# SyncE's loads of the prologue and of block 0, each queued behind the landing of an earlier load

## What is computed

```python
# q, k, v: (4, 8, 576, 64); pooled by 4 along the sequence, and a band of +-3
q_d = q.reshape(B, H, Sd, factor, D).mean(axis=3)          # k_d, v_d likewise
out_up = np.repeat(sm_attn(q_d, k_d, v_d), factor, axis=2)
mask = np.abs(pos[:, None] - pos[None, :]) < factor
out_local = softmax(where(mask, scale * q @ k.T, -1e9)) @ v
x = (out_up + out_local)     # as 2304 tokens x 512
h = x @ w_in                 # w_in: 512 x 2048
g = h * np.tanh(log1p(exp(h)))
out = g @ w_out              # w_out: 2048 x 512
```

## Time and profile before

| | us |
|---|---|
| three timed runs | 510.19, 510.17, 505.64 |
| their median | 510.17 |
| the profiled execution | 505.87 |
| its span, first to last instruction | 504.1 |
| busy in it: PE | 487.2 (97%) |
| DVE, ACT, POOL | 219.1, 176.0, 121.2 |
| moved by DMA | 35.01 MB |

### The profile page before, as it was taken

One profiled execution on the slowest core, in us unless ns is written; L12 is line 12 of the kernel. 1 busy time (PEld: TensorE's weight loads), 2 busy tenths in 40 slices (PEclk: granted clock), 3 DMA queues, 4 the chain that ended last, 5 costly groups with the idle time before them and its releaser, 6 DMA issues.

```text
span 504.1 us, 9597 instructions
## 1 busy us (share of the span) xinstructions
PE 487.2 (97%) x4040; PEld 434.7 (86%) x4040; DVE 219.1 (43%) x390; ACT 176.0 (35%) x399; POOL 121.2 (24%) x164
## 2 busy tenths in 40 slices
PE   7789999999999999899999989999999999999997
PEld 7678888988999988788898978989899998999996
DVE  5845875665322234536356363644222222232221
ACT  4664865462211123534353452534121111211111
POOL 3997546524100003134141322412000000000000
PEclk9989999999999999999999999999999999999999
DMA  8995522131200001503213051220010000100001
GB/s 283 334 315 160 203 74 59 48 106 34 89 1 0 1 2 47 169 1 106 59 48 105 3 168 37 70 59 1 1 62 1 0 1 0 44 21 1 0 2 62
DMA packets 15836, 35.01 MB, mean 69 GB/s; under 512 B 1840, under 2 KB 1968, under 8 KB 15792
## 3 DMA queue, kind: packets, MB, share of 16 engines
q1 hardware_dynamic: 15792, 34.38, 21.5%
HBM read 29.66 MB, written 4.72 MB: 68 GB/s over the span
## 4 chain that ended last, share of the span: by engine, by line
PE 86%; issue 3%; DVE 3%; ACT 3%; DMA 2%; POOL 2%; SPq 0%; ACTq 0%; POOLq 0%; DVEq 0%
PE acc L600 38%; PE hidden L583 36%; PE att L478 2%; PE att L491 2%; PE att L537 2%; PE att L507 1%; PE att L544 1%; PE att L519 1%; DMA k_t<-in_k 1%; DMA out<-stage 1%; POOL prob L381 1%; DMA v_win<-in_v_win 1%; POOL prob_pool L389 1%; DVE x_low L802 1%; PE hidden L537 1%
## 5 line engine op out<-in xcount | busy, mean ns | idle before, releaser
L814 DVE CAST g_high<-hidden 128x384 fp32r<-128x384 f32 x96 | 53.4, 557 | 205.3 <-PE acc L600 160.0
L583 PE MATMUL hidden<-x_high,w_in_high 128*128 128x384 f32 x384 | 130.2, 339 | 0.5 <-DVE g_low L816 0.5
L583 PE MATMUL hidden<-x_high,w_in_low 128*128 128x384 f32 x384 | 129.4, 337 | 0.0
L583 PE MATMUL hidden<-x_low,w_in_high 128*128 128x384 f32 x384 | 128.9, 336 | 0.0
L1006 ACT ACTIVATE hidden<-hidden 128x384 f32<-128x384 f32 x96 | 45.7, 476 | 234.2 <-PE hidden L583 233.9
L600 PE MATMUL acc<-w_out_high,g_high 128*128 128x512 f32 x288 | 115.0, 399 | 0.0
L600 PE MATMUL acc<-w_out_high,g_low 128*128 128x512 f32 x288 | 113.4, 394 | 0.0
L600 PE MATMUL acc<-w_out_low,g_high 128*128 128x512 f32 x288 | 113.3, 393 | 0.0
L583 PEld LDWEIGHTS hidden<-x_high,w_in_high 128*128 128x128 f32 x384 | 72.1, 188 | 4.8 <-DVE g_low L816 0.8
L583 PEld LDWEIGHTS hidden<-x_low,w_in_high 128*128 128x128 f32 x384 | 72.1, 188 | 3.1
L583 PEld LDWEIGHTS hidden<-x_high,w_in_low 128*128 128x128 f32 x384 | 72.0, 188 | 0.0
(11 more groups left out here) (93 smaller groups left out, 452.6 us busy)
## 6 DMA issues: line engine op xcount, KB each, us to landing
v_win<-in_v_win SPq DMA_DIRECT2D x16, 384.0 KB, 4.2
v_in<-in_v SPq DMA_DIRECT2D x16, 320.0 KB, 3.6
k_t<-in_k SPq DMA_DIRECT2D x16, 292.0 KB, 3.8
q_t<-in_q SPq DMA_DIRECT2D x16, 288.0 KB, 2.8
out<-stage SPq DMA_DIRECT2D x17, 256.0 KB, 2.1
w_in_raw<-in_w_in SPq DMA_DIRECT2D x16, 256.0 KB, 12.5
w_out_raw<-in_w_out SPq DMA_DIRECT2D x16, 256.0 KB, 5.0
out<-last_stage SPq DMA_DIRECT2D x1, 256.0 KB, 2.1
```

The lines of the kernel that those rows point to most:

```text
L583: last = nc.tensor.matmul(hidden[:, g % HB, 0:TB], w, x[:, k, cols], start=(k == 0 and i == 0), stop=(k == KT - 1 and i == 2))
L814: nc.vector.tensor_copy(g_high[:, g % GB], x).then_inc(g_rounded, 1)
```

## The change

SyncE's list in the prologue and in block 0 keeps its loads and their order. Between them now stand waits for earlier loads: most issues wait until the load three places ahead of it has landed (a load_qk or a load_v counting as one), so that three or four calls are under way at a time. From w_in(7) on it is the load three pieces back. The rest of SyncE's list and all other engines' lists are as they were.

```diff
--- before.py
+++ after.py
@@ -286,25 +286,43 @@
                 sp.dma_start(const[:], const_l).then_inc(const_loaded, 16)
                 load_w_in(0)
                 load_qk(0)
+                sp.wait_ge(const_loaded, 16)
                 load_w_in(1)
+                sp.wait_ge(w_in_loaded[0], 16)
                 load_w_out(0)
+                sp.wait_ge(qk_loaded[0], 32)
                 load_qk(1)
+                sp.wait_ge(w_out_loaded[0], 16)
                 load_qk(2)
+                sp.wait_ge(qk_loaded[1], 32)
                 load_w_in(2)
+                sp.wait_ge(qk_loaded[2], 32)
                 load_v(0)
+                sp.wait_ge(w_in_loaded[2], 16)
                 load_v(1)
+                sp.wait_ge(v_loaded[0], 32)
                 load_qk(3)
+                sp.wait_ge(v_loaded[1], 32)
                 load_w_in(3)
                 load_w_in(4)
+                sp.wait_ge(qk_loaded[3], 32)
                 load_qk(4)
+                sp.wait_ge(w_in_loaded[3], 16)
                 load_w_in(5)
+                sp.wait_ge(w_in_loaded[4], 16)
                 load_w_out(1)
+                sp.wait_ge(qk_loaded[0], 64)
                 load_v(2)
+                sp.wait_ge(w_in_loaded[5], 16)
                 load_w_out(2)
+                sp.wait_ge(v_loaded[2], 32)
                 load_v(3)
+                sp.wait_ge(w_out_loaded[2], 16)
                 load_v(4)
+                sp.wait_ge(v_loaded[3], 32)
                 load_w_in(6)
                 for f in range(7, FT):
+                    sp.wait_ge(w_in_loaded[f - 3], 16)
                     load_w_in(f)
                 sp.wait_ge(out_ready, AHEAD)
                 for f in range(EARLY_OUT, 6):
```

## The result

| | before | after |
|---|---|---|
| timed runs | 9 | 9 |
| median, us | 508.40 | 512.48 |
| lowest and highest, us | 505.64, 510.97 | 511.69, 514.84 |
| profiled execution, us | 505.87 | 512.26 |
| its span | 504.1 | 510.5 |

The ratio of after to before is 1.0086, with a 95% interval of 1.0053 to 1.0119. The change made the kernel slower, by 0.5 to 1.2%. The forecast was 503.3 us and its range ended at 510.3: the sign was wrong and the time lies outside the range.

A forecast was written before the change was run, and what follows sets the result against it. Before 41.15 us the prologue, a chain through all engines, was taken as the bound, then PE itself. Late loads +0.4, stalls -0.7 and -1.6, clock -0.6 gave -2.5 us; added to the profiled 505.87: 503.3 us, range 501.6 to 510.3.

The forecast's parts named there:

- The step that failed: SyncE's list: the waits delay only further loads; w_in(15) goes out at about 41 us, w_out(3) at 41.4.
- (a): Prologue: loads issued later, qk(1), v(0) and qk(3) close to their consumers; POOL passes on +0.4 us (bounds 0 and 1.2).
- (b): Prologue: PE's code refills find a short queue, both "issue" stalls (1.69 and 1.31 us) go: -0.7 and -1.6 us.
- The rule weighed in the prediction: Code refills: DMA engines alternate queues packet by packet, so a shorter backlog gives nothing: 506.3 us.
- The prediction's own rule: Code refills at PE's block ends: the refill lets all queued loads pass, 0.7 MB meaning 2 us of transfer.
- piece of fixed size: Rival 1's reason: the refill stands behind a fixed-size piece of the queue, which four loads may still fill.
- The clock, -0.6 us: Prologue, 35 to 40 us: without PE's stalls the clock does not fall; -0.6 us, 0 if it falls anyway.
- The sum: At outputs(3): +0.4 - 0.7 - 1.6 - 0.6 = -2.5 us, start 37.15 instead of 39.65, kept to the end.
- Rival 3: Prologue, starved queue: qk(1), v(0), qk(3) land late, POOL passes on about 1.5 us, clock falls, 1.0; 508.4 us; chance 0.10.
- Rival 4: Prologue: the clock falls nowhere and the first stall is worth its full 1.69 us: 502.3 us; chance 0.07.
- Rival 1: Prologue: refills wait as long as before, only late loads count: 506.3 us, or 510.6 beside higher runs; chance 0.20.
- Rival 2: Whole kernel: the gain is made, but runs stay at the higher level: 510.2 - 2.5 = 507.7 us; chance 0.23.

The follow-up runs named there:

- e12: Before with only the load of qk(5) moved from behind w_out(5) to behind w_out(15), no wait added: 513.91 us, ratio 1.0129 to before.
- e10: e7 plus two early waits, for qk(0) ahead of w_in(2) and for qk(1) ahead of v(1): 505.67 us, ratio 0.9953 to before.
- e8: Before with its loads in e7's order by need, but without any added wait: 507.95 us, ratio 1.0001 to before.
- e9: After with its 17 single waits, w_in(10) to w_in(15) moved behind w_out(3) and around qk(5): 508.46 us, ratio 1.0022 to before.
- e1: After without the nine waits in the loop over w_in(7) to w_in(15): 509.39 us, ratio 1.0027 to before.
- e5: After with all its waits, only qk(5) moved ahead of w_out(3) to w_out(5): 509.52 us, ratio 1.0044 to before.
- e3: After without its first seven waits, so loads up to v(1) issue freely: 512.67 us, ratio 1.0088 to before.
- e2: Before plus only the nine waits in the loop over w_in(7) to w_in(15): 508.31 us, ratio 1.0000 to before.
- e7: Before with loads reordered by need, free up to v(1), then waits for the load two or three back: 504.65 us, ratio 0.9943 to before.
- e4: Before plus only after's first seven waits, up to v(1): 508.07 us, ratio 1.0002 to before.
- e6: Before with each load waiting for the landing six calls back, where after mostly takes three: 506.72 us, ratio 0.9988 to before.

## Why the prediction was wrong, step by step

**The step that failed.** "Queued behind SyncE's waits are only further loads; w_in(15) now goes out at about 41 us, and w_out(3) right behind it, at 41.4 instead of 41.3". w_in(15) went out at 47.56 and w_out(3) at 47.94. Two things were wrong in it. First the time: each wait was priced at an idle queue's landing (3.1 to 3.8 us) only where a consumer stood close behind it, and the rest of the list was taken to keep up. In the trace the waits stand in series. Predicted and measured landings drift apart: k(1) 10.1 to 10.3 and 10.7; qk(2) 11.6 and 13.3; v(0) 15.9 and 17.9; qk(3) 20.2 and 21.6; qk(4) 23.5 and 27.1; v(2) 27.7 and 32.6; v(3) 32 and 37.3; w_in(6) 35 and 41.5. Second, "only further loads": one of them, qk(5), had a time by which it was wanted. The prediction looked for consumers of late loads up to ACT and w_out(3) and stopped there. A row of before already had POOL idle for 2.75 us in front of this very load, and what stood behind it had hardly any slack: POOL waited another 0.24 us (for DVE) before prob(4), and PE took prob(4) without a gap. The prediction names no row of POOL past 41 us.

**"From there on PE is bound by itself ... so the 2.5 us stay to the end"** was wrong for the same reason. PE was 98% busy after 41.15, but pair 4's and pair 5's chains run under block 0, and they were just in time. e12 shows it without any wait added: 5 us of a load's landing, 7 us of time. Over the kernels of the table b0 stays at 84 us while k(5) is 8.7 or less. Where the block ran at a clock of 1.00, it grows from there by about 1 us for each (e10: 9.6 and 85.56; e8: 9.7 and 84.83; e9: 10.0 and 85.24; e1: 11.2 and 86.92; e5: 12.2 and 87.83), and PE's gap ahead of pair 4's turn grows with it (0.47, 0.56, 0.88, 2.56, 3.22 us). After, e3 and e12 lie above that by the clock's part. e2 and e7 don't belong to the row: no gap, and the clock made both numbers.

**(a) The late loads, +0.4 us** for qk(1), v(0) and qk(3): e4 has the seven waits that make qk(1) and v(0) late, alone, and gives 1.0002; qk(3) landed at 21.6, and POOL took it at 22.26 without waiting. The median shows no such cost, though it can't tell 0.4 us from nothing. POOL's wait for k_t(1) was 1.73 us, as forecast. What was left out is qk(2): pool_q(2) stands ahead of prob(0) in POOL's list, and PE waited 1.40 us for prob(0) instead of 0.66. Beside it v(2), which the prediction gave 1 us of room, landed 4.9 us later than it said; PE lost 1.15 us for it. PE's timeline of after, and POOL's ahead of it:

```profile
34.88 1.23 PE L562 MATMUL hidden<-prob_pool_t,v_pool 72*64 72x144 f32 x8 [1.15 <-POOL v_pool L393]
```
```profile
32.63 0.72 POOL L390 TENSOR_TENSOR v_pool<-v_in 72x256 f32<-72x256 f32 x1 [1.93 <-DMA v_win<-in_v_win]
```

**(b) The stalls, -0.7 and -1.6 us.** Right as far as the stalls go. After has no gap put down to "issue" at the two block ends where before had 1.69 and 1.31 us; only that before outputs(3), 0.59 us, is left, as in before (0.73). e7 against e8 measures the term with all that hangs on it, the clock too: 3.3 us.

**Why the refill is sooner.** At the block end of about 440 (439 instructions had started by 21.16 in after) the refill packet came at about 23.8. Windows of after up to that block end, and the DMA queues of after from 23.7 to 23.9:

```profile
0.00:21.16 21.16, 16.51 (x219) 15.09 (x220) 11.44 (x28) 10.22 (x28) 10.90 (x22) 0.92 0.78 242
```
```profile
q8 instruction: 1, 0.02, 30.5%
```

That is 2.6 us, with three loads of 0.8 MB not yet landed. Counted in the same way before's wait is 4.7 us, with 3.6 MB (the prediction's 4.3 takes the block end 0.4 us too late), and at the later block end with nothing queued 0.6 (the prediction's 0.3). The rule weighed in the prediction ("DMA: Bandwidth & Descriptors" of the Trainium skill, queues, rings and completion order: each engine takes turns between its queues, packet by packet) would have the refill wait for no backlog; the runs speak against it, 0.6 us with nothing queued, 0.9 to 3.6 us with 0.7 to 0.9 MB (after, e7), 3.9 to 6.2 us with 2 MB and more (both profiles of before, e6, e8). The prediction's own rule, that all of the backlog has to pass, is no better at the upper end: 2.0 MB (e6) gave 4.03 us and 3.8 MB (before) 5.51. That is nearer to the rival's "piece of fixed size", except that four loads do not fill it: after's waits are shorter, and its stalls are gone.

**The clock, -0.6 us.** Wrong. From 32 to 41 us the granted clock of after is 0.65, as before's 0.66 from 35 to 40, and it was 0.50 from 18 to 21 us as well (0.88 over the prologue). PE stood still before the first fall for POOL (1.40 us for prob(0), until 17.75) and before the second for POOL's v_pool(2) (1.15 us, until 34.88), rather than for its code. But after's waits don't force this: with the same seventeen waits e9, e5 and e1 ran the prologue at 1.00 and took 40.42 to 41.55 us.

**The sum.** The -2.5 us at outputs(3) didn't come. The forecast put outputs(3) at 37.15, before had it at 39.65, and PE's timeline of after has it here:

```profile
42.26 0.91 PE L555 MATMUL acc<-prob_t,v_win 54*64 54x48 f32 x48 [0.59 <-issue]
```

With the same seventeen waits and the clock at 1.00 it came at 39.71 (e1), 39.02 (e5) and 38.93 (e9), against 39.65 and 41.09 in the two profiles of before. So the stalls' gain was there but smaller than 2.5 us, since PE waited longer for prob(0) and for v(2), and in after's profile the clock took more than all of it. Why after's clock is lower than theirs stays open.

Block 0 adds 3.5 us in the profiles, for the late qk(5): 2.1 of idle time and 1.4 of busy time at the lower clock behind the gap. How much of the 4.1 us between the medians is qk(5) alone is not settled. e1 and e5 keep the gap (2.56 and 3.22 us) and lie only 1.1 and 1.5 us above before. But the clock alone doesn't make the loss either: 66 runs of before, made beside the experiments, had a mean granted clock of 0.987 to 0.993, and the slowest took 510.62 us; the eight runs of after in that range took 511.69 to 514.84.

In the prediction's own figures, the forecast's lower bound of 502.2 doesn't follow from the bounds named beside it (late loads at 0 instead of +0.4 give 503.0), and the sum was added to 505.87, the profile's time, where the median of nine runs is 508.4.

**The rivals.** Rival 3, the starved queue, had the right sign and roughly the right sentence ("each issued only when an earlier one has landed"), but its place was wrong: it looked at qk(1), v(0) and qk(3), none of which cost a time that can be measured, and it would be decided "once qk(1) lands after about 11 us"; qk(1) landed at 10.7. Its fall of the clock behind a wait of PE is in after's profile (0.50 from 18 to 21 us), but not in those of e1, e5 and e9 with the same waits. Rival 4, a clock that falls nowhere, is not what after's runs show: their mean granted clock is 0.983 to 0.993. Rival 1 (the refill waits as before) falls with e7 and e8. Rival 2 was right in one point: the runs of before at 510 exist, and the nine runs' median is 508.4, not the 505.9 of the profile to which the sum was added.

## What to carry to other kernels

A queue's issuing engine is a list like any other: a wait in it delays everything behind it, so follow the last load that the list still has to issue to the time when it is wanted, and look there for an engine that already waits for it (here POOL, idle for 2.75 us in front of k_t(5)). Throttling loads by "wait for the third one back" puts landings in series into that list (after's w_in(6) to w_in(15) took from 37.31 to 47.56 to go out, e1's from 38.44 to 43.54); what paid here was ordering the loads by the time they are wanted together with waits only where the queue would otherwise hold megabytes (e7, ratio 0.9943, where the order alone gave 1.0001 and after's waits alone 1.0086). And a bound engine that is 98% busy is not yet safe from a chain that runs beneath it without slack.

## What the runs showed of the hardware

- The wait of an instruction refill behind the loads under way was 0.6 us with none, 0.9 to 3.6 with 0.7 to 0.9 MB, 4.0 with 2 MB, and 3.9 to 6.2 us with 2.6 to 4 MB, where it no longer grew with the amount. PE went on 1.3 to 1.5 us after the packet's end wherever it was held by it.
- The load of k_t(5), 292 KB, took 3.1 to 3.7 us where one or two other loads had not landed at its issue (both profiles of before, e2, e4, e6, e7), 4.6 to 5.4 with three to five (e5, e8, e9, e10, after) and 5.7 to 6.4 with six to nine (e1, e3, e12). What is issued just ahead of a load that is wanted matters as much as its own issue time.
- The scatter of 2 to 5 us between runs of one kernel goes in part with the granted clock: e5's five runs with a mean of 0.997 or 1.00 took 508.12 to 509.57 us, its five with 0.989 to 0.993 took 509.46 to 513.92; e7's six at 1.00 took 502.97 to 504.97, its four others 504.36 to 506.58. Of before's runs beside the experiments the 48 at 0.993 have a median of 507.1 us, the six at 0.987 one of 510.0; the 15 at 0.997, with 508.0, don't fit in. No run of after was above 0.993.
